# Attention stage of a three-stage kernel: experts chosen for two groups at a time, biases made on GpSimd, state kept head by head

## What is computed

```python
# 1: gated linear attention, per batch and head, token after token
f = 1 / (1 + exp(-f_logit))                     # (4, 8, 768, 48)
state = f[t][:, None] * state + outer(k[t], v[t])   # 48 x 48
y[t] = q[t] @ state
# 2: one expert of 8 for each token, weighted by its probability
logits = x @ w_gate + modality_bias[modality_id]; e = argmax(logits)
out[token] = softmax(logits)[e] * (relu(x[token] @ w1[e]) @ w2[e])   # 384 -> 1024 -> 384
# 3: normalised gated MLP
xn = x / rms(x) * rms_g
out = (silu(xn @ w_gate) * (xn @ w_val)) @ w_out                     # 384 -> 1536 -> 384
```

## Time and profile before

| | |
|---|---|
| median of 3 runs | 860.37 us (860.11 to 860.67) |
| profiled execution | 857.94 us, span 856.2 us |
| attention (to the meeting at L256) | 0 to 150.2 us |
| experts and the MLP | 152.2 us to the end |
| PE busy in the whole span | 821.0 us, 96% |
| DVE, ACT, POOL busy | 471.3, 385.9, 127.4 us |

### The profile page before, as it was taken

The page is one execution under the profiler, slowest core; times in us unless marked ns, Lnnn a source line. Parts: engine busy times, 40 slices in busy tenths (PEclk is TensorE's granted clock), DMA queues, the critical chain, the costliest instruction groups (busy, mean ns, idle before and its releaser), DMA issues.

```text
span 856.2 us, 15107 instructions
## 1 busy us (share of the span) xinstructions
PE 821.0 (96%) x5300; PEld 750.8 (88%) x5300; DVE 471.3 (55%) x782; ACT 385.9 (45%) x742; POOL 127.4 (15%) x143
## 2 busy tenths in 40 slices
PE   6899997789999999989999999999999999999997
PEld 6788886779999999989888888888888888888887
DVE  8999997778767666643544343343334334333332
ACT  5888886455665555553323312331231223123112
POOL 3012113248444000010000200100020010001001
PEclk9999999999999999999999999999999999999999
DMA  9877756698987787732000100200020000000000
GB/s 190 175 157 181 169 133 240 224 364 251 306 257 244 263 319 268 243 98 71 22 1 14 61 1 1 73 0 0 0 73 0 0 37 0 0 0 37 0 0 37
DMA packets 44086, 96.54 MB, mean 113 GB/s; under 512 B 9168, under 2 KB 25040, under 8 KB 43920
## 3 DMA queue, kind: packets, MB, share of 16 engines
q1 hardware_dynamic: 39952, 85.81, 34.2%
q0 software_dynamic: 3840, 9.47, 3.1%
q10 hardware_dynamic: 256, 0.79, 0.3%
HBM read 76.75 MB, written 19.29 MB: 112 GB/s over the span
## 4 chain that ended last, share of the span: by engine, by line
PE 78%; issue 2%; DVE 1%; DMA 1%; SPq 0%; POOL 0%; ACT 0%; DVEq 0%; ACTq 0%
PE h_ps L1771 16%; PE h_ps L1773 16%; PE h_ps L1772 16%; PE ym_ps L1771 7%; PE ym_ps L1773 7%; PE ym_ps L1772 7%; PE xTm_ps L1772 3%; PE xTm_ps L1771 3%; PE xTm_ps L1773 3%; PE xT_ps L1788 1%; PE xTm_ps L1779 1%; DMA w_in<-in_w 1%; POOL out L1434 0%; ACT w_hi L1452 0%; SPq L1292 0%
## 5 line engine op out<-in xcount | busy, mean ns | idle before, releaser
L1746 DVE TENSOR_TENSOR gs<-h_ps,sig 128x512 f32<-128x512 f32 x72 | 49.8, 691 | 176.2 <-ACT sig L1546 176.2
L1546 ACT ACTIVATE sig<-h_ps 128x512 f32<-128x512 f32 x72 | 43.1, 598 | 159.5 <-PE h_ps L1773 159.5
L1557 ACT CAST h_hi<-hid 128x512 fp32r<-128x512 f32 x72 | 44.6, 620 | 149.6 <-DVE hid L1749 149.6
L1771 PE MATMUL h_ps<-x_hi,w_hi 128*128 128x256 f32 x312 | 89.3, 286 | 7.2 <-DVEq L1673 3.8
L1773 PE MATMUL h_ps<-x_lo,w_hi 128*128 128x256 f32 x312 | 89.2, 286 | 0.0
L1772 PE MATMUL h_ps<-x_hi,w_lo 128*128 128x256 f32 x312 | 89.0, 285 | 0.0
L1771 PE MATMUL h_ps<-w_hi,wg_hi 128*128 128x512 f32 x216 | 85.5, 396 | 0.0
L1773 PE MATMUL h_ps<-w_lo,wg_hi 128*128 128x512 f32 x216 | 84.6, 392 | 0.0
L1773 PE MATMUL h_ps<-w_lo,wv_hi 128*128 128x512 f32 x216 | 84.2, 390 | 0.0
L1771 PE MATMUL h_ps<-w_hi,wv_hi 128*128 128x512 f32 x216 | 84.0, 389 | 0.0
L1772 PE MATMUL h_ps<-w_hi,wv_lo 128*128 128x512 f32 x216 | 84.0, 389 | 0.0
(11 more groups left out here) (231 smaller groups left out, 1831.1 us busy)
## 6 DMA issues: line engine op xcount, KB each, us to landing
w_raw<-in_w SPq DMA_DIRECT2D x52, 384.0 KB, 5.1
w_in<-in_w SPq DMA_DIRECT2D x52, 384.0 KB, 5.4
qkf_in<-in_qkf SPq DMA_DIRECT2D x43, 288.0 KB, 5.0
y_sorted<-x_group SPq DMA_DIRECT2D x13, 384.0 KB, 3.4
v_in<-in_v SPq DMA_DIRECT2D x24, 192.0 KB, 4.6
x_regions<-zero_row SPq DMA_DIRECT2D x12, 384.0 KB, 3.4
x_group<-x_regions SPq DMA_DIRECT2D x12, 384.0 KB, 3.9
g_in<-in_wg SPq DMA_DIRECT2D x3, 768.0 KB, 7.7
```

Source lines behind the costliest of these rows:

```text
L1546: nc.scalar.activation(sig[:], g_ps, ACT.Sigmoid).then_inc(sig_done, 1)
L1557: nc.scalar.copy(h2_hi[:, fb % HELD], hid[:]).then_inc(h2_hi_done, 1)
L1746: nc.vector.tensor_tensor(gs[:], g_ps, sig[:], ALU.mult).then_inc(gs_done, 1)
L1771: nc.tensor.matmul(out, hi, rhs_hi, start=first, stop=False)
```

## The change

- **PE:** `ds` becomes eight matmuls, one a head: weights of 64 or 48 columns, 48 moving columns. The state's part of y becomes eight matmuls on 48 x 48, on partitions 0 to 47 or 64 to 111. The start-up matmuls are 20 and go round four parts of their bank.
- **State:** `state` and `grown` are stored without the other head's empty half (128x4x48 instead of 128x4x128). `grown` is one DVE instruction on 112 partitions; ACT's four `state` instructions have 48 columns each.
- **Routing:** three batches, (groups 0 and 1), (2 and 3), (4), chosen in steps 10, 18 and 22 and placed in steps 12, 20 and 24. Instructions of the first two have twice the columns. `x_tiles` is a ring of 10 tiles; POOL's scatters of a batch follow each other after `place`, four of the first and second batch waiting for `x_kept` of later tiles.
- **GpSimd** makes `token_bias` after its constants; DVE no longer fills `grown`, and fills `yT_ps` after the first scans. SP issues the loads of the gate, modality and bias after five constants instead of seven.

```diff
+BATCHES = ((0, 2 * B), (2, 2 * B), (4, B));  SLOTS = 10;  LATE = 12
 # DVE
-                    for r, d in ((0, 0), (PAD, D)):
-                        ds = ds_ps[:, 0:DM].rearrange("p (j e) -> p j e", j=PR)
-                        last = nc.vector.tensor_tensor(grown[r:r + D, s, :, r:r + D], ds[r:r + D, :, d:d + D],
-                                                       state[r:r + D, s, :, r:r + D], ALU.add)
+                    nc.vector.tensor_tensor(grown[0:ROWS, s], ds[0:ROWS], state[0:ROWS, s], ALU.add).then_inc(grown_done, 1)
...
-            nc.vector.memset(grown[:], 0.0).then_inc(filled, 1)
-            nc.vector.memset(yT_ps[:], 0.0).then_inc(yT_zero, 1)
-            dve.wait_ge(filled, 4)
+            dve.wait_ge(filled, 3)
             for b in range(FIRST_TWO):
                 sums(0, b, b)
-            dve.wait_ge(consts, CONSTS)
+            nc.vector.memset(yT_ps[:], 0.0).then_inc(filled, 1)
+            dve.wait_ge(consts, 4)
 # PE
                 for j in range(PR):
-                    mm = nc.tensor.matmul(ds_ps[0:ROWS, 2 * D * j:2 * D * (j + 1)], ks[:, s, j, 0:ROWS],
-                                          v_in[:, s, 2 * D * j:2 * D * (j + 1)], start=True, stop=True)
+                    for par in range(2):
+                        h, r, end = 2 * j + par, PAD * par, ROWS if par else PAD
+                        mm = nc.tensor.matmul(ds[r:end, j], ks[:, s, j, r:end], v_in[:, s, D * h:D * (h + 1)],
+                                              start=True, stop=True)
...
-                        nc.tensor.matmul(acc[0:ROWS, j], state[0:ROWS, s, j, 0:ROWS], qT[0:ROWS, s, j], start=(j == 0), stop=False,
+                        for r in (0, PAD):
+                            nc.tensor.matmul(acc[r:r + D, j], state[r:r + D, s, j], qT[r:r + D, s, j], start=(j == 0), stop=False,
 # ACT
+                    if n >= SLOTS:
+                        before = n - SLOTS
+                        if before < LATE:
+                            act.wait_ge(scattered[before % B], 16 * (before // B + 1))
+                        else:
+                            act.wait_ge(scattered_late, 16 * B)
+                    nc.scalar.copy(rt.x[:, n % SLOTS, :].rearrange("p (j r) -> p j r", j=PR), ...
 # POOL
+            token_bias()
+            for i, (g0, w) in enumerate(BATCHES):
+                pool.wait_ge(marks, (i + 1) * Routing.PLACED)
+                for n in range(g0 * B, g0 * B + w):
+                    if B <= n < LATE:
+                        pool.wait_ge(x_kept, n - B + SLOTS + 1)
+                    rt.scatter(nc, n, x_regions).then_inc(...)
```

More of the change, by code:

```diff
@@ L76, in __init__, with by_expert, by_token, choose @@
         self.before = sb("before", [P, P])
[L77 to L82, removed]
+        self.restart = sb("restart", [P, 2 * B * E])
+        self.restart_one = sb("restart_one", [P, B * E])
+        self.biased = sb("biased", [P, 2 * B * E])
+        self.most = sb("most", [P, 2 * B])
+        self.first = sb("first", [P, 2 * B])
+        self.chosen = sb("chosen", [P, E * 2 * B])
+        self.upto = sb("upto", [P, E * 2 * B])
         self.shift = sb("shift", [P, E])
-        self.rows = sb("rows", [P, E, B])
-        self.row_f = sb("row_f", [P, B])
-        self.row = [sb(f"row{h}", [P, B], U32) for h in range(2)]
+        self.rows = sb("rows", [P, E * 2 * B])
+        self.row_f = sb("row_f", [P, 2 * B])
+        self.row = sb("row_of", [P, NT], U32)
         self.chosen_all = sb("chosen_all", [P, CH, E, B])
         self.row_all = sb("row_all", [P, CH, B])
-        self.x = sb("x_group", [P, 2, B, DM])
-    def choose(self, nc, dve, c, marks, count):
+        self.x = sb("x_tiles", [P, SLOTS, DM])
+    def by_expert(self, a, w):
+        return a[:, 0:E * w].rearrange("p (e b) -> p e b", b=w)
+    def by_token(self, a, w):
+        return a[:, 0:E * w].rearrange("p (b e) -> p b e", e=E)
+    def choose(self, nc, dve, c, w, marks, count):
         def step(k, ins):
@@ L114, in choose @@
[L114 to L121, removed]
+            return a[:, 0:w].rearrange("p (b o) -> p b o", o=1).broadcast_to([P, w, E])
@@ new lines, in choose @@
+        tiles = bass.ds(c * B, w)
+        biased, chosen = self.by_token(self.biased, w), self.by_expert(self.chosen, w)
+        restart = self.restart if w > B else self.restart_one
+        step(1, nc.vector.tensor_tensor(biased, self.logits[:, tiles, :], self.token_bias[:, tiles, :], ALU.add))
+        step(2, nc.vector.tensor_reduce(self.most[:, 0:w], biased, AX.X, ALU.max))
+        step(3, nc.vector.tensor_tensor(biased, biased, per_token(self.most), ALU.is_equal))
+        rank = self.rank_e[:].rearrange("p (o e) -> p o e", o=1).broadcast_to([P, w, E])
@@ L123, in step, with count, place @@
+    def count(self, nc, w, pre_ps, cnt_ps):
+        last = self.by_expert(self.upto, w)[:, :, w - 1]
+        nc.tensor.matmul(pre_ps, self.before[:], last, start=True, stop=True)
+        return nc.tensor.matmul(cnt_ps, self.ones_r[:], last, start=True, stop=True)
+    def place(self, nc, dve, c, w, to, pre_ps, cnt_ps, marks, count):
         def step(k, ins):
@@ L536, in step @@
                     for j in range(PR):
-                        last = nc.scalar.activation(state[:, s, j], grown[:, s, j], ACT.Copy,
-                                                    scale=fade[:, s, j:j + 1])
+                        last = nc.scalar.activation(state[0:ROWS, s, j], grown[0:ROWS, s, j], ACT.Copy,
+                                                    scale=fade[0:ROWS, s, j:j + 1])
                     last.then_inc(state_done, 1)
@@ L693, in _ @@
             pe.wait_ge(consts, 4)
-            for _ in range(START_WARM_UP):
-                nc.tensor.matmul(ks_ps[:, 0], tri[:], tri[:], start=True, stop=True)
+            for i in range(START_WARM_UP):
+                nc.tensor.matmul(ks_ps[:, i % PR], tri[:], tri[:], start=True, stop=True)
             def growth(s, n):
```

188 lines of the change are left out of this document (92 added, 96 removed).

## The result

| | before | after |
|---|---|---|
| median, runs side by side | 860.52 us (860.11 to 861.4) | 855.77 us (854.24 to 856.03) |
| profiled execution, span | 857.94, 856.2 us | 856.03, 854.3 us |
| `kT` of tile 0, 3, 6 starts | 12.30, 22.68, 39.47 | 10.12, 22.30, 36.12 |
| `kT` of tile 20 | 117.91 | 112.12 |
| meeting at the block's end | 150.1 | 146.3 |

The ratio is 0.9946, 95% interval 0.9926 to 0.9966: faster by 0.5%. The forecast was 857.5.

What follows compares the result with a forecast made beforehand. PE was taken to pace plain steps at 5.37 us, with DVE paying for routing from slack. Gains of 3.4 at tile 20 and 0.3, less 0.8, gave 2.9 us: 860.37 becomes 857.5, range 851.5 to 863.

Steps and rivals of the forecast that it cites:

- Start: First scans to first `kT`: without DVE's fill of `grown`, `kT` comes at about 10.1 instead of 12.30, gain 2.2 us.
- the bound that I named with 0.8: At the start, the arrival of tile 2 could take back 0.8 us; none was counted.
- Steps 0 to 5: DVE-paced early steps: token bias off DVE gains 1.5 us, `grown` as one instruction 1.4 over four steps.
- Steps 6 to 19: PE-paced steps to `kT` of tile 20: step 5.65 instead of 5.37 us, 80.1 against 78.4, 1.7 us lost.
- rival 2: PE's step gets shorter, 5.0 to 5.4 us, by cheaper shape changes or `ds`; 852.6 us at 5.3; chance 0.22.
- The counts: Routing steps before tile 20: PE waited 3.3 us over three before; one now (step 12), at 0.5.
- The ring: Step 13: ACT's copy of tile 10 waits 1.6 us for tile 0's scatter; 0.5 reaches PE (0 to 2.6).
- Step 20 to the end: Tile 20 to the meeting: `grown` gains 0.3, eight scatters crowding DMA lose 0.8 (gain 1.2 to loss 1.8).
- Rival 3: End pile-up: `x_ahead`, queued on SP behind weights and v beside more scatters, eats the gain; 860 us; chance 0.17.
- Rival 1: State reads of two heads take turns on one PSUM bank; step 6.7 us, 870 (868 to 873); chance 0.10.
- The row's price of a load: PE weight loads: 121 ns for 128 columns in the trace (0.97 / 8), where the skill page has 107.

Runs made afterwards that it cites:

- warm: The changed kernel with 24 instead of 20 start-up matmuls and 5 and 4 unread matmuls in steps 1 and 2; 0.995 of before.
- start_warm: The kernel before with the change's start edits, 24 instead of 22 start-up matmuls and 5 and 4 unread matmuls in steps 1 and 2; 0.9982 of before.
- the start's part alone: The kernel before with biases and the fill of `grown` on GpSimd, `yT_ps` filled behind the first scans, gate loads earlier; 1.0013 of before.
- ring12: The changed kernel with 12 instead of 10 places for x and five instead of four scatter semaphores; 0.9938 of before.
- v_first: The changed kernel with the loads of v for tiles 22 and 23 issued ahead of the expert's weights; 0.9957 of before.
- one_group: The changed kernel with experts chosen one group at a time again, in five batches; 0.992 of before.
- the state's part alone: The kernel before with only the change's edits to `ks`, `state`, `grown`, `ds` and the read; 854.82 us beside 860.32.
- old_ds: The changed kernel with `ds` as before, `grown` in two instructions and its fill on GpSimd; 866.06 us, 1.0056 of before.
- best: The changed kernel with five one-group batches plus 24 start-up matmuls and the unread matmuls in steps 1 and 2; 851.82 us beside 860.32.

## Why the prediction was right, and where its terms were not

The sign was right and the time is in the range; 857.5 was 1.7 us high. At the meeting the forecast's gain was 2.9, the profiled one is 3.8. That it came so near is in part luck, since the terms are off by more, in both directions: the gain at tile 6 is 3.35 where I had 5.1, from there to tile 20 it is +2.4 where I had -1.7, and from there to the meeting -2.0 where I had -0.5.

- *Start, 2.2.* First `kT` at 10.12: right. What it was worth was not: the gain is 2.2 at tile 0, 1.3 at tiles 1 and 2, and 0.38 at tile 3. The first loss is the bound that I named with 0.8 and counted as nothing: DVE now waits 0.81 for the load of tile 2. Through ACT that wait also lengthens PE's idle time before its second `ks` from 0.48 to 1.37. The second loss, 0.9, comes with the half clock, for which the forecast has no term. warm and start_warm keep the clock: at tile 6 that is worth 0.5 us beside after, and 1.1 beside the start's part alone.
- *Steps 0 to 5.* From tile 3 to tile 6 the gain is 2.97; the token bias and three `grown` were 1.5 + 3 x 0.36 = 2.6: right.
- *Steps 6 to 19, a loss of 1.7.* This step failed, with its sign. Measured: a gain of 2.4, 76.0 against 78.4 us. The mis-sized terms: `ds` at 0.83 is 0.54, and two borders at 0.21 each are 0.18 and, behind `ds`, 0.13. I priced loads and borders by the scores' part, the nearest in the shape of its weights. But its matmuls move 128 columns and those of `ds` 48. The two groups that move 128, the read and the scores' part, both take 0.82, with weights of 48 and of 128 rows; that the moving columns set this pace fits all the rows, and no run here tests it by itself. The single records add that in `ds` the two column halves load side by side (58 and 45 ns a load), so that the eight of 64 columns alone fill the 0.54 (7 x 58 ns and the last load's 138). The step is 5.31: rival 2's condition holds (5.0 to 5.4, chance 0.22), though its time, 852.6, was not reached. The counts were priced at 0.5 and cost 0.2 in all.
- *The ring, 0.5 (0 to 2.6).* The mechanism was right and the size low: ACT waits 2.94, and 1.5 us reach tile 20 (ring12). The scatter of tile 0 took at least 4.7 us to land where I used the median of 4.1, and the 2 us that I gave PE before it needs `yT` weren't there: its loads for `x` stood idle 1.60.
- *Step 20 to the end, a loss of 0.5.* It was 2.0: 34.2 us from tile 20 to the meeting against 32.2 before. Rival 3 named the place and half the mechanism (the queue on SP and the scatters), but not the load of v, for which PE now waits 3.4 us, nor the clock that follows. It decides 2 us, not all of the gain. In v_first the stretch is 32.7, so by this one trace the late v accounts for 1.5, and PE then waits 1.58 for `x_ahead`, which stands behind it; one_group, with four scatters fewer ahead of `x_ahead`, takes 3.4 off this stretch.
- *Rival 1, serial reads.* Dead: sixteen loads of the read last 0.82, the next group starts 0.19 later, and the matmuls of the two heads start 7 ns apart, though all write the one bank of `yT_ps`. (Its terms, 14 us less 2.9 and 1 more on 860.4, add up to 872 to 873; the 870 given for it was a slip.) The rule of the Trainium skill that I set beside it (TensorEngine Tiling (Array Packing), Gotcha 1: PSUM Pressure) doesn't hold for these two heads, which differ in both rows and columns of the array.
- *The row's price of a load.* My 121 ns for 128 columns is a group's time divided by its loads, and so holds the whole length of the last one. The single records of `x` start 112 ns apart.
- *The two parts of the change.* I ascribed most of the gain to the start and a loss to the state. The runs say the opposite: the state's part alone is 0.9928, the start's alone 1.0013.

Open: how much of the end's loss is the clock, how much the ring's second wait and how much the queue. ring12 leaves the eight scatters and has the clock at 1.00 from 128 to 140 us, and takes 33.3, but it drops the ring's wait as well and had part of its half clock before 128 (0.91 from 110 to 128). Open is also why start_warm's gain of 2.4 us at tile 20 isn't seen at its meeting.

## What to carry to other kernels

Price a matmul group whose shape changes from all its neighbours: its loads, and each border by the pair of shapes that meet there; the group nearest in weights missed by a third, most likely because it moved more columns. Bringing work forward pays only if its inputs come as early and the engines behind it stay busy: where TensorE gets new idle time in a thin stretch, read its granted clock there, and fill the gap with matmuls that nobody reads if it fell. Batching small steps moves their transfers together, so look at which later load stands behind them in a queue before counting what the batching saves.

## What the runs showed of the hardware

- Sixteen loads of 64 and 48 columns in turn took 0.54 us, where eight of 112 took 0.87. The loads of 64 columns started 58 ns apart and, beside them on the other half of the array, those of 48 columns 45 ns apart. The Trainium skill's rule (TensorE: Matmul & The Clock Gate, LDWEIGHTS) gives 0.75 for the sixteen one after another, an estimate from the page; the trace doesn't agree. Sixteen of 48 columns under matmuls of 128 moving columns took 0.82, whether they cover 128 rows or 48.
- The price of a change of shape depends on the pair: 0.10 from whole to column halves, 0.05 from there to quarters, 0.18 from quarters to the scores' part, 0.09 from whole to quarters (old_ds).
- Two heads on different rows and columns of the array wrote one PSUM bank with their matmuls side by side: these started 7 ns apart, and the next two 109 ns later (128 moving columns each).
- The clock fell to 1.2 GHz behind two idle times of 1.4 us near the start, for some 7 us. It stayed at 2.4 GHz in warm (one of 0.88), in v_first (0.77 and 1.44, with the same start code as after) and before (2.24 and 0.48).
- The last two loads of v landed 8.2 us after their issue before, 11.0 to 11.2 with eight scatters beside them (after, ring12), 9.3 with four (one_group), and 2.5 to 3.2 when issued ahead of the expert's weights (v_first).
- An indirect scatter takes 2.6 to 7.2 us to land, with a median of 4.6 where eight go out together and 3.4 in best, where they are spread.
